# Causal masks of attention added into the key bias by GpSimd instead of by TensorE products

## What is computed

```python
scores = scale * np.matmul(q, k.transpose(0, 1, 3, 2))        # 2 x 8 x 576 x 576
causal = np.triu(np.ones((S, S), dtype=bool), k=1)
cum = np.cumsum(np.maximum(s, 0.0), axis=-1)
bias = -(cum[:, :, :, None] - cum[:, :, None, :])
scores = np.where(causal, -1000000000.0, scores + np.minimum(bias, 0.0))
scores = scores - np.max(scores, axis=-1, keepdims=True)
attn = np.exp(scores)
attn = attn / (np.sum(attn, axis=-1, keepdims=True) + 1e-09)
return np.matmul(attn, v)
```

## Time and profile before

| | |
|---|---|
| time, median of 3 runs | 1081.54 us (1081.49 to 1081.89) |
| time of the profiled execution | 1081.88 us |
| its span | 1080.1 us |
| attention, with the start of the experts in its last part | about the first 110 us |
| a period of attention, steady | 11.47 us |
| PE busy over the span | 1073.8 us, 99% |
| DVE, ACT, POOL busy over the span | 65%, 39%, 31% |
| mean granted clock of PE | 0.998 of 2.4 GHz |

### The profile page before, as it was taken

One profiled execution on the slowest core, in us unless ns is written; L12 is line 12 of the kernel. 1 busy time (PEld: TensorE's weight loads), 2 busy tenths in 40 slices (PEclk: granted clock), 3 DMA queues, 4 the chain that ended last, 5 costly groups with the idle time before them and its releaser, 6 DMA issues.

```text
span 1080.1 us, 19243 instructions
## 1 busy us (share of the span) xinstructions
PE 1073.8 (99%) x6746; PEld 969.3 (90%) x6746; DVE 705.0 (65%) x1497; ACT 425.4 (39%) x984; POOL 336.7 (31%) x441
## 2 busy tenths in 40 slices
PE   9999999999999999999999999999999999999999
PEld 7777989899898998989899898989989899898997
DVE  7778966566574666657566564756656697586682
ACT  6888637143241523325152341614234433132230
POOL 1446604132140412214041231404223375144420
PEclk9999999999999999999999999999999999999999
DMA  8862111101111111121111111111212002102002
GB/s 184 196 141 71 59 40 40 56 26 57 59 39 39 39 58 37 41 58 39 39 39 58 39 45 52 39 39 39 59 40 59 21 21 79 40 21 77 22 1 88
DMA packets 91702, 59.27 MB, mean 55 GB/s; under 512 B 32736, under 2 KB 78048, under 8 KB 91648
## 3 DMA queue, kind: packets, MB, share of 16 engines
q1 hardware_dynamic: 90416, 58.23, 19.1%
q10 hardware_dynamic: 1232, 0.33, 0.2%
HBM read 56.15 MB, written 2.40 MB: 54 GB/s over the span
## 4 chain that ended last, share of the span: by engine, by line
PE 98%; DVE 1%; ACT 1%; issue 0%; POOL 0%; DVEq 0%
PE bank L1783 15%; PE bank L1785 15%; PE bank L1784 15%; PE bank L1912 14%; PE bank L1914 14%; PE bank L1913 14%; PE bank L1731 2%; PE bank L1768 2%; PE bank L1662 2%; PE bank L1618 1%; PE bank L1702 0%; PE bank L1809 0%; PE bank L1791 0%; DVE kept_c L1264 0%; PE bank L1743 0%; PE bank L1942 0%
## 5 line engine op out<-in xcount | busy, mean ns | idle before, releaser
L701 POOL TENSOR_TENSOR hl<-kept_c,hh 128x320 fp32r<-128x320 f32 (+1 forms) x128 | 104.9, 820 | 525.1 <-ACT kept_c L901 525.1
L1912 PE MATMUL bank<-w2h,hh 128*128 128x512 f32 x680 | 266.6, 392 | 0.0
L1914 PE MATMUL bank<-w2h,hl 128*128 128x512 f32 x680 | 265.1, 390 | 0.0
L1913 PE MATMUL bank<-w2l,hh 128*128 128x512 f32 x680 | 265.1, 390 | 0.0
L1432 DVE SCALAR_TENSOR_TENSOR acc<-bank,P,acc 128x512 f32<-128x512 f32 x135 | 101.3, 751 | 196.1 <-PE bank L1914 196.1
L1783 PE MATMUL bank<-xh,w1h 128*128 128x320 f32 (+1 forms) x704 | 210.1, 298 | 1.0 <-DVE kept_c L1264 0.9
L1264 DVE TENSOR_TENSOR kept_c<-bank,kept_c 128x256 f32<-128x256 f32 (+1 forms) x440 | 183.8, 453 | 38.3 <-PE bank L1785 34.9
L1785 PE MATMUL bank<-xh,w1l 128*128 128x320 f32 (+1 forms) x704 | 208.7, 296 | 0.0
L1784 PE MATMUL bank<-xl,w1h 128*128 128x320 f32 (+1 forms) x704 | 208.6, 296 | 0.0
L899 ACT ACTIVATE hh<-kept_c 128x256 fp32r<-128x256 f32 (+1 forms) x256 | 113.1, 443 | 155.7 <-DVE kept_c L1264 155.7
L798 ACT ACTIVATE kept_one<-bank 128x256 f32<-128x256 f32 (+1 forms) x88 | 34.8, 395 | 322.7 <-PE bank L1785 322.6
(11 more groups left out here) (155 smaller groups left out, 1420.7 us busy)
## 6 DMA issues: line engine op xcount, KB each, us to landing
raw<-in_moe_w SPq DMA_DIRECT2D x32, 512.0 KB, 3.6
raw<-in_moe_w SPq DMA_DIRECT2D x32, 256.0 KB, 2.7
raw<-in_moe_w SPq DMA_DIRECT2D x64, 128.0 KB, 2.7
bias<-cum_dram SPq DMA_DIRECT2D x14, 256.0 KB, 3.6
raw<-in_moe_w_a SPq DMA_DIRECT2D x12, 256.0 KB, 2.9
raw<-in_moe_w_b SPq DMA_DIRECT2D x24, 128.0 KB, 2.9
raw<-in_moe_w_out SPq DMA_DIRECT2D x6, 512.0 KB, 3.9
bias_tail<-cum_dram SPq DMA_DIRECT2D x16, 144.0 KB, 4.2
```

Source lines behind the costliest of these rows:

```text
L701: pool.tensor_tensor(hl[:, 3 - place, columns(b, s)], src[:, 0:width(s)], hh[:, place, columns(b, s)].bitcast(F32), ALU.subtract).then_inc ...
L1912: pe.matmul(bank, hh[:, place, at], w2h[:, place, :], start=(nth == 0), stop=False)
L1913: pe.matmul(bank, hh[:, place, at], w2l[:, place, :], start=False, stop=False)
L1914: ins = pe.matmul(bank, hl[:, 3 - place, at], w2h[:, place, :], start=False, stop=(nth == 3))
```

## The change

For the pairs 1 to 7 ("from the third head on") the masks are no longer TensorE products. The key bias of a head in SBUF is now eight blocks of 128: block 0 holds keys of block 0, blocks 2 to 5 hold the keys of blocks 0 to 3, and blocks 1, 6 and 7 are made by GpSimd as the diagonal blocks of the tiles 0, 2 and 1: the keys of blocks 0, 2 and 1 plus `maskb`. Block 5 gets the mask in place, for tile 3. So each tile finds its keys in blocks at one stride: (1), (2, 7), (0, 3, 6), (2, 3, 4, 5). The mask of the tail is added in place to the last 64 columns of `bias_tail`. VectorE's instructions read the same number of columns as before, through a pattern of blocks.

- **Added on SyncE**: in `load_bias(p)`, p > 0, one DMA of 64 KB for each head, 2 a pair, between the loads of `bias` and of `bias_tail`; 14 in all.
- **Added on GpSimd**: `mask_bias(k+1)` in period k, seven instructions (two of 2 x 128 columns, four of 128, one of 64). It waits for all six DMAs of pair k+1, and stands behind `spread_tail_queries(k)` and ahead of `wide_reciprocals(k-1)`.
- **Removed on TensorE**: 9 products for each of 7 pairs, 63. `sc_mm` is told by the last score product.
- **VectorE** waits for `bias_masked` (both steps of GpSimd) where it waited for the DMAs.

The odd pairs' bias lies in a part of `xh` that is not yet used.

```diff
             if p > 0:
                 for r in range(2):
-                    sp.dma_start(bias[z][:, r, :],
-                                 cum_ap[2 * p + r:2 * p + r + 1, 0:MAIN].broadcast_to([PART, MAIN])).then_inc(bias_loaded[z], DMA)
+                    row = cum_ap[2 * p + r:2 * p + r + 1, :]
+                    sp.dma_start(bias_of(z, r)[:, FIRST_KEYS:FIRST_KEYS + MAIN],
+                                 row[:, 0:MAIN].broadcast_to([PART, MAIN])).then_inc(bias_loaded[z], DMA)
+                    sp.dma_start(bias_of(z, r)[:, 0:PART],
+                                 row[:, 0:PART].broadcast_to([PART, PART])).then_inc(bias_loaded[z], DMA)
...
+        def mask_bias(p):
+            if not (present(p) and p > 0):
+                return
+            z = p % 2
+            pool.wait_ge(bias_loaded[z], DMA * loads_of_bias(p))
+            mask = maskb[:, :].rearrange("p (o s) -> p o s", o=1)
+            for r in range(2):
+                blocks = bias_blocks(z, r)
+                pool.tensor_tensor(blocks[:, 1:8:6, :], blocks[:, 2:4, :], mask.broadcast_to([PART, 2, PART]), ALU.add)
+                pool.tensor_tensor(blocks[:, 6, :], blocks[:, 4, :], maskb[:, :], ALU.add)
+                ins = pool.tensor_tensor(blocks[:, 5, :], blocks[:, 5, :], maskb[:, :], ALU.add)
+            ins.then_inc(bias_masked, 1)
+            pool.tensor_tensor(bias_tail[z][:, MAIN:S], bias_tail[z][:, MAIN:S], maskt[:, :],
+                               ALU.add).then_inc(bias_masked, 1)
...
         for k in PERIODS:
             spread_tail_queries(k)
+            mask_bias(k + 1)
             wide_reciprocals(k - 1)
...
             elif (t, r) == (0, 1):
                 at_least(dve, pt_mm, 8 * (p - 1))
-                dve.wait_ge(bias_loaded[z], DMA * (4 * (p // 2 + 1) - (2 if z == 0 else 0)))
+                dve.wait_ge(bias_masked, 2 * p)
...
         def score_masks(p, g):
-            if not present(p):
+            if p != 0:
                 return
```

More of the change, by code:

```diff
@@ L62, in attention_experts_product @@
     GROUPS = FP // PART // GC
+    BIAS_BLOCKS = 8
     PARTS = [(0, SPLIT), (SPLIT, S)]
@@ L139, in attention_experts_product @@
     recips, _ = sb("recips", [PART, 2, 9], F32)
-    qk, nat, bias, bd, bias_tail, scores, scores_tail, vt, spread = ([None] * 2 for _ in range(9))
+    qk, nat, bd, bias_tail, scores, scores_tail, vt, spread = ([None] * 2 for _ in range(8))
     qk[0], at = sb("qk_0", [PART, 2, 2, S], F32R, slot_at[1])
@@ L150, in attention_experts_product @@
     at = tl_end - 2 * 2 * S * 4
-    for z in range(2):
-        bias[z], at = sb(f"bias_{z}", [PART, 2, MAIN], F32, at)
+    bias_0, at = sb("bias_0", [PART, 2, BIAS_BLOCKS * PART], F32, at)
     bd[0], at = sb("bd_0", [PART, 2, PART], F32R, at)
@@ L158, in attention_experts_product, with bias_of, bias_blocks @@
     assert at <= hh_at + N * 4
+    last_features = (B * KC - 2) * S * 4
+    bias_1 = [sb("bias_1_0", [PART, BIAS_BLOCKS * PART], F32, 16512 + last_features)[0],
+              sb("bias_1_1", [PART, BIAS_BLOCKS * PART], F32, 16512 + B * KC * S * 4 + last_features)[0]]
+    assert BIAS_BLOCKS * PART <= 2 * S
+    def bias_of(z, r):
+        return bias_0[:, r, :] if z == 0 else bias_1[r][:, :]
+    def bias_blocks(z, r):
+        return bias_of(z, r).rearrange("p (n s) -> p n s", s=PART)
     pT_at = at
@@ L224, in attention_experts_product @@
     v_loaded = [sem(f"v_loaded{z}") for z in range(2)]
+    bias_masked = sem("bias_masked")
     bias_loaded = [sem(f"bias_loaded{z}") for z in range(2)]
@@ L410, in attention_experts_product, with loads_of_bias @@
     RING_PLACE = {unit: n for n, unit in enumerate(RING)}
+    FIRST_KEYS = 2 * PART
+    TILE_BLOCKS = [slice(1, 2), slice(2, 8, 5), slice(0, 7, 3), slice(2, 6)]
+    def loads_of_bias(p):
+        return 6 * (p // 2 + 1) - (4 if p % 2 == 0 else 0)
     UNIT_NTH = {5: 1, 2: 2, 7: 3, 1: 4, 4: 5, 3: 6, 6: 7, 0: 8}
@@ L866, in first_bias_rows @@
                 act.wait_ge(first_bias_mm, half + 1)
-                copy(bias[0][:, :, half * SPLIT:(half + 1) * SPLIT],
+                copy(bias_0[:, :, FIRST_KEYS + half * SPLIT:FIRST_KEYS + (half + 1) * SPLIT],
                      FIRST_BIAS[half][:, :].rearrange("p (r s) -> p r s", r=2), first_bias)
@@ L1177, in biased @@
                 at_least(dve, pt_mm, 8 * (p - 1))
-                dve.wait_ge(bias_loaded[z], DMA * (4 * (p // 2 + 1) - (2 if z == 0 else 0)))
-            dve.tensor_tensor_reduce(scores[z][:, r, COL[t]:COL[t + 1]], bank[:, col:col + n], bias[z][:, r, 0:n],
-                                     -1.0 / INV, 3.0e38, ALU.add, ALU.min, neg_max[:, z, c:c + 1]).then_inc(sc_done, 1)
+                dve.wait_ge(bias_masked, 2 * p)
+            blocks = slice(2, 2 + t + 1) if p == 0 else TILE_BLOCKS[t]
+            dve.tensor_tensor_reduce(scores[z][:, r, COL[t]:COL[t + 1]].rearrange("p (n s) -> p n s", s=PART),
+                                     bank[:, col:col + n].rearrange("p (n s) -> p n s", s=PART),
+                                     bias_blocks(z, r)[:, blocks, :], -1.0 / INV, 3.0e38, ALU.add, ALU.min, neg_max[:, z, c:c + 1]).then_inc(sc_done, 1)
         def biased_tail(p, half):
@@ L1661, in score_products @@
                         rows = slice(r * D, (r + 1) * D)
-                        pe.matmul(S_BANK[first + r][:, col:col + n], qk[z][rows, a, 0, t * PART:(t + 1) * PART],
-                                  qk[z][rows, b, 1, 0:n], start=(nth == 0 and i == 0), stop=False)
+                        ins = pe.matmul(S_BANK[first + r][:, col:col + n], qk[z][rows, a, 0, t * PART:(t + 1) * PART],
+                                        qk[z][rows, b, 1, 0:n], start=(nth == 0 and i == 0),
+                                        stop=(p > 0 and nth == len(tiles) - 1 and i == 2))
+            if p > 0:
+                ins.then_inc(sc_mm, 1)
         def score_masks(p, g):
-            if not present(p):
+            if p != 0:
                 return
@@ L1703, in score_tail @@
                                 qk[z][:, b, 1, half * HALF:(half + 1) * HALF], start=(i == 0),
-                                stop=(i == 2 and half == 0))
-            if half == 1:
+                                stop=(i == 2 and (half == 0 or p > 0)))
+            if half == 1 and p == 0:
                 ins = pe.matmul(S_BANK[3][:, MAIN - HALF:HALF], identb[:, :], maskt[:, :], start=False, stop=True)
```

## The result

| | before | after |
|---|---|---|
| median of 4 runs each, same chip | 1081.72 us (1081.49 to 1081.94) | 1100.23 us (1100.19 to 1100.35) |
| span of the profiled execution | 1080.1 us | 1098.4 us |
| mean granted clock of PE | 0.998 | 0.992 |

The ratio after to before is **1.0174** (95%: 1.0162 to 1.0187): the change costs 18.5 us. The forecast was 9.1 us, and 1100.2 lies above the range, which ended at 1096.5. The direction came out as predicted, the size is double.

The account below looks back on a forecast made before the run. PE was taken to bound the kernel; late DMA landings, POOL's masks and wide copies would delay spread_recips, moving period 7's from 93.12 to 102.2: +9.1 us on 1081.88, less 0.34 for the median, 1090.6 us; range 1085.5 to 1096.5.

Parts of the forecast that it names:

- E1: Start of spread_recips on PE in period 1: put at 29.35 us, against 24.26 before.
- E1 to S3: From spread_recips in period 1 to the first bias issue in period 3: 14.12 us less 0.48 of masks, 13.64.
- E3 to S5: From spread_recips in period 3 (54.85) to the first bias issue in period 5 (68.5), by the 13.64 us step.
- E5 to E6: From spread_recips in period 5 (79.65) to that in period 6 (91.05), the latter set with a landing of 4.5 us.
- E6 to E7: From spread_recips in period 6 (91.05) to that in period 7 (102.2): 11.51 us before, less 0.33 of masks.
- saving on PE: Mask products of pairs 1 to 7 leave PE's path: 0.48 us a period, 3.4 us over seven pairs.
- period of 10.99: Attention period on PE without mask products: 11.47 less 0.48 us, where PE alone sets the pace.
- rival 3: POOL's 4.23 us gap takes the masks in whole and PE saves 3.4 us: 1078.1 us; chance 0.05.
- S + 6.4: Landing of period 5's second tail load after the first bias issue: 1.5 plus 0.8 to issue, 4.1 to land.
- The seven instructions of a pair: POOL's masks for one pair: 3.7 us, with bounds of 2.3 and 5 us.
- main case: The wait chain at spread_recips as worked out, without a falling clock: +9.1 us, 1090.6 us; chance 0.73.
- Rival 1: The wait chain, with PE's clock falling to half after its waits: +1.5 to +4.5 us, 1092 to 1095; chance 0.13.

Follow-up runs that it names:

- e3: The kernel before with the mask products of pairs 1 to 7 left out and nothing in their place; 1077.85 us, ratio 0.9971.
- e1: The changed kernel with one line moved: GpSimd makes the masks of pair k+1 behind the wide reciprocals of pair k-1; 1083.52 us, ratio 1.0024.
- e8: The kernel before plus the 14 loads and new layout, GpSimd waiting for them ahead of the wide reciprocals but making no masks; 1089.67 us, ratio 1.0077.
- e9: The changed kernel without its 14 additional loads, block 0 keeping zeros, masks and wait in place; 1090.42 us, ratio 1.0084.
- e4: The changed kernel with useless TensorE products just ahead of spread_recips in periods 1, 3 and 5; 1096.84 us, ratio 1.0143.
- e5: The changed kernel with six of GpSimd's seven mask instructions of a pair left out, only the tail's mask made; 1092.05 us, ratio 1.0102.
- e7: The kernel before with only the 14 added loads and the bias's new place, masks as TensorE products, no wait on GpSimd; 1082.41 us, ratio 1.0014.
- e2: The changed kernel with masks behind the wide reciprocals and pair 1's masks kept as TensorE products; 1081.72 us, ratio 1.0004.

## Why the prediction was right in direction and short in size

Adding up along the same chain as the forecast, with its own points (E: start of `spread_recips`, S: first bias issue):

| step | forecast | measured | difference |
|---|---|---|---|
| E1 | 29.35 | 32.04 | +2.69 |
| E1 to S3 | 13.64 | 15.99 | +2.35 |
| S3 to E3 | 11.85 | 11.90 | +0.05 |
| E3 to S5 | 13.65 | 15.40 | +1.75 |
| S5 to E5 | 11.15 | 12.33 | +1.18 |
| E5 to E6 | 11.40 | 12.63 | +1.23 |
| E6 to E7 | 11.15 | 11.24 | +0.09 |

The sum is 9.34, the whole excess (111.53 against 102.2).

**Right.** The saving on PE (3.4 us; e3 shows 3.1 by the ratio), the period of 10.99, the place of the wait and its cause, its repetition every second period, and that POOL's idle time is no room when the data is not there. Moving the wait (e1) and adding it alone (e8) show it from both sides. DVE's blocked reads cost nothing that shows: e1's period is 10.99 us with them. Period 7, 11.24 us, is as forecast. For rival 3 to win, masks and wide copies would have had to be done 8.4 us after S; in period 3 they were done at 59.8, 11.7 after S. The signs that the prediction named came out larger than it had them: waits of 5.87, 3.50 and 3.65 us (some 4, and between 2 and 3), first bias issues 12.1 to 16.8 us apart (12 to 13), and 13.2 us as the mean period between E1 and E7 (12.1).

**Mis-sized: when the data is there.** The step "S + 6.4" and its like in period 1 took landings from the kernel before and gave the two added loads only their 0.8 us of issue. Measured: in period 1 the second tail load was issued at 21.7 instead of 20.6 and landed 6.0 us later instead of 4.0, so POOL began 3.2 us late. (S itself was 18.40 and not 17.14: SP's issues of the keys ahead of it took 1.80 and 1.36 us.) In period 5 it landed 5.7 us after its issue and not 4.1, and from S to the start of the masks it was 8.1 instead of 6.4. In period 3, 7.7 against 7.1. These are 5.5 us in all. Without the added loads (e9) the data came much as the rows of before say: the masks started at 23.77 in period 1 (19.8 + 4.0), and 5.9 and 5.7 us after S in the periods 3 and 5 (1.5 + 4.8 and 1.5 + 4.1). So the error is what two more loads do to the queue. The range held a longest landing of 5.6 in the periods 3 to 6 but only 4.3 in period 1, and no later issue.

**Mis-sized the other way: the masks.** The seven instructions of a pair took 3.04 us (55.71 to 58.75) and not 3.7; with the copies and the release, from the start of the masks to `spread_recips`, it was 4.2 and not 4.75 us in each of three periods: 1.6 us given back, so that 3.9 of the 5.5 are left in the sum. The Trainium skill, "GPSIMD Engine Reference" (3.1 Elementwise), by whose 2.2 ns a column they were put at an estimated 2.4 us, was under the measured time by as much as the forecast was over; the rows below give the slope as 1.9 ns a column and a fixed part of some 0.18 us that the page's one length can't show.

**The step that failed: the clock, which the main case put at nothing.** Rival 1 stood at 0.13, priced at +1.5 to +4.5 us, because PE had kept full clock where it was busy for 0.76 of a microsecond. That row was the wrong neighbour: it shows a wait of 0.24 us, not of 4. Nor was the fall from 9 to 11 us a neighbour: the prediction says that PE had run small products with waits between, but PE's timeline of before has no wait from 1.30 to 14 us. No row of before shows a wait of 4 us, so nothing spoke for leaving the clock out. It fell at all three waits, and the three steps that follow a wait (E1 to S3, E3 to S5, E5 to E6) are 5.3 us longer, about what the products themselves lost there (2.2, 1.7 and 1.6 us). Kept up, the clock brings at least 3.4 (e4). The Trainium skill, "TensorE: Matmul & The Clock Gate" (HAM oscillation), describes a kernel that waits for data in every round of its loop and loses its clock at each of these waits; the trace of after agrees, three times of three.

By the sum, neither error alone makes the miss: 1090.6 + 5.3 is 1095.9 and 1090.6 + 3.9 is 1094.5, both inside the range. Together they leave it.

**Costs multiply here.** The two errors were also taken as alternatives, the longer landing inside the main case and the clock as a rival to it. But a later landing lengthens PE's wait, and the longer wait brings the half clock, which delays the next S. Without the loads (e9) the waits are shorter and the clock falls once; without the mask work (e5) as well. So the shares don't add up to 18.5: loads alone 0.9 us, wait alone 7.3 on top, the loads in place 9.8, six of seven mask instructions in place 8.2, the clock at least 3.4.

## What to carry to other kernels

Before work is put into an engine's idle time, ask what it waits for and what stands behind it in that engine's order: a wait for a DMA ahead of something that TensorE needs costs more than the work itself, and exchanging two lines can give nearly all of it back. Take the landing of a load from a profile in which the queue carries the added bytes, or add a microsecond to it, and let SP's issue slip too. When the sum gives TensorE waits like those seen here (3 to 6 us), put the time at half clock behind each such wait into the main case, not into a rival.

## What the runs showed of the hardware

- **Loads beside loads.** Two loads of 64 KB more in a row of four moved the median landing of a period's tail loads from between 3.8 and 5.0 us (periods 1 to 6 of before; four of them in the earlier trace rows) to between 4.9 and 5.7. Where they were left out again (e9) it was 4.0 to 5.0.
- **SP's issue.** An issue that takes 0.34 to 0.6 us lasted 1.3 to 2.4 us where it stood behind a long row of others (18.40 and e2's 29.44 above); that the row is the cause is not shown.
- **The clock behind waits.** PE's waits of 5.87, 4.19, 3.65, 3.63, 3.50 and 2.98 us each had a clock of 0.50 from their end or at most 1.4 us later, in after's first wait and in e9 already within it; behind those of 2.39 us (e5, period 4), 1.76, 1.69 and less it did not fall. Two waits of 1.91 and 2.37 us with 4 us between their ends (e1, period 1) were followed by it as well. A fall needs no wait: in before the clock was 0.50 from 10 to 13 us with PE busy all along, in about half of the executions (14 of 25 beside e1 to e4 had a mean clock below 1.000), and it cost 1.2 us (1081.96 against 1080.81).
- **POOL.** Two-operand additions with one operand in bf16 took 0.67 us for 256 columns, 0.42 for 128 and 0.30 for 64, while one on two float operands took 0.74 for 256 in before.
